# mLSTM attention with a mixture of experts: fades spread by a product and an exponential instead of a stored copy and transfers

## What is computed

```
m_new = max(f_gate[t] + m, i_gate[t])
f = exp(f_gate[t] + m - m_new);  i = exp(i_gate[t] - m_new);  m = m_new
C = f * C + i * outer(v[t], k[t]);   n = f * n + i * k[t]
y[t] = sigmoid(o_gate[t]) * (C @ q[t]) / max(|n . q[t]|, 1)
```

## Time and profile before

| | us |
|---|---|
| median of three runs (407.35 to 410.41) | 407.49 |
| the profiled execution, measured from outside | 407.79 |
| its span, from the first to the last instruction | 406.1 |
| TensorE busy | 374.9 |
| VectorE busy | 238.7 |
| ScalarE busy | 220.7 |
| GpSimd busy | 78.6 |

### The profile page before, as it was taken

The page is one execution under the profiler, slowest core; times in us unless marked ns, Lnnn a source line. Parts: engine busy times, 40 slices in busy tenths (PEclk is TensorE's granted clock), DMA queues, the critical chain, the costliest instruction groups (busy, mean ns, idle before and its releaser), DMA issues.

```text
span 406.1 us, 9533 instructions
## 1 busy us (share of the span) xinstructions
PE 374.9 (92%) x3484; PEld 315.6 (78%) x3484; DVE 238.7 (59%) x556; ACT 220.7 (54%) x436; POOL 78.6 (19%) x119
## 2 busy tenths in 40 slices
PE   2989978898799879999999999999999999999996
PEld 2667756576667657634569999999999999999996
DVE  8745756745856576441158756556556556556553
ACT  3554546455546565312048866666666666666662
POOL 4255645354544544000000000000000000000000
PEclk9996999998989999999999999999999999999999
DMA  6389999999999998996900001001001001001001
GB/s 179 90 245 254 268 283 254 243 263 265 260 260 241 254 257 283 350 363 217 364 6 2 0 2 65 2 2 65 0 0 65 0 0 65 0 0 65 0 2 65
DMA packets 31816, 56.83 MB, mean 140 GB/s; under 512 B 3524, under 2 KB 20548, under 8 KB 31524
## 3 DMA queue, kind: packets, MB, share of 16 engines
q1 hardware_dynamic: 28308, 45.84, 40.5%
q10 hardware_dynamic: 3472, 10.51, 9.6%
HBM read 51.83 MB, written 4.42 MB: 139 GB/s over the span
## 4 chain that ended last, share of the span: by engine, by line
PE 68%; DMA 13%; SPq 11%; DVE 4%; issue 2%; ACT 1%; ACTq 0%; DVEq 0%
DMA row_x<-cum_scratch 12%; PE heads_banks L1109 7%; PE high_banks L1111 7%; PE high_banks L1110 7%; PE high_banks L1109 7%; PE heads_banks L1110 7%; PE heads_banks L1111 7%; PE low_banks L1097 5%; SPq L393 3%; PE low_banks L1032 2%; PE heads_banks L823 2%; PE low_banks L802 2%; PE low_banks L1013 2%; PE low_banks L959 2%; SPq L351 2%
## 5 line engine op out<-in xcount | busy, mean ns | idle before, releaser
L747 ACT ACTIVATE relu_h<-low_banks 128x512 f32<-128x512 f32 x96 | 57.4, 598 | 60.5 <-PE low_banks L1097 60.1
L1422 DVE CAST sq_hi<-sq_h 128x512 fp32r<-128x512 f32 x96 | 41.0, 427 | 66.7 <-ACT sq_h L752 66.1
L1424 DVE TENSOR_TENSOR sq_lo<-sq_h,sq_hi 128x512 fp32r<-128x512 f32 x96 | 66.5, 692 | 3.3
L752 ACT ACTIVATE sq_h<-relu_h 128x512 f32<-128x512 f32 x96 | 60.6, 632 | 3.1
L1111 PE MATMUL high_banks<-wo_hi,sq_lo 128*128 128x320 f32 x192 | 59.3, 309 | 0.0
L1109 PE MATMUL high_banks<-wo_hi,sq_hi 128*128 128x320 f32 x192 | 59.3, 309 | 0.0
L1110 PE MATMUL high_banks<-wo_lo,sq_hi 128*128 128x320 f32 x192 | 59.3, 309 | 0.0
L1109 PE MATMUL heads_banks<-wo_hi,sq_hi 128*128 128x320 f32 x192 | 59.3, 309 | 0.0
L1110 PE MATMUL heads_banks<-wo_lo,sq_hi 128*128 128x320 f32 x192 | 59.1, 308 | 0.0
L1111 PE MATMUL heads_banks<-wo_hi,sq_lo 128*128 128x320 f32 x192 | 59.1, 308 | 0.0
L1152 DVE TENSOR_TENSOR att_w<-low_banks,att_w 128x512 f32<-128x512 f32 x48 | 30.9, 685 | 37.2 <-POOL att_w L538 21.0
(11 more groups left out here) (177 smaller groups left out, 548.8 us busy)
## 6 DMA issues: line engine op xcount, KB each, us to landing
w_sb<-in_w SPq DMA_DIRECT2D x8, 1280.0 KB, 12.5
w_a<-in_w ACTq DMA_DIRECT2D x16, 512.0 KB, 9.6
kv_in<-in_kv SPq DMA_DIRECT2D x24, 320.0 KB, 13.8
qk_in<-in_qk SPq DMA_DIRECT2D x24, 256.0 KB, 7.2
fade_b<-fade_scratch SPq DMA_DIRECT2D x40, 128.0 KB, 8.3
o_in<-in_o_gate SPq DMA_DIRECT2D x24, 160.0 KB, 13.6
out<-out_sb SPq DMA_DIRECT2D x5, 640.0 KB, 3.2
wo_raw<-in_w_out SPq DMA_DIRECT2D x4, 640.0 KB, 12.0
```

The source lines that it names most:

```text
L747: act.activation(relu_h[:, slot], bank[slot][:, :], ACT.Relu).then_inc(relu_done, 1)
L752: act.activation(sq_h[:, slot], relu_h[:, slot], ACT.Square).then_inc(sq_done, 1)
L1422: dve.tensor_copy(sq_hi[:, slot], sq_h[:, slot]).then_inc(hi_done, 1)
L1424: dve.tensor_tensor(sq_lo[:, slot], sq_h[:, slot], sq_hi[:, slot].bitcast(F32), ALU.subtract).then_inc(lo_done, 1)
```

## The change

The fades are no longer stored and loaded. A constant matrix `cum_pick` (42 x 128, zeros and ones) is made at the start by GpSimd with a memset and two selects. In each step, `spread_fade` on TensorE multiplies it with the 42 rows of `row_x`: it picks the high and the low row of `cum` for each group of heads and writes their sum to the 64 partitions of the group, 4 x 128 values each, in bank 1. `raise_fade` on ScalarE takes the exponential from there into `fade_b`. The readers wait for `fade_ready` in place of a transfer. Because bank 1 is used once more, the second decay product and `logit` wait for the exponential, and `spread_fade` waits for the decay exponentials of its step. `load_rows` also waits until the product four steps back has read its row. On GpSimd `mask` now stands ahead of `scale_q`. The exponential at the start, its tile and the scratch tensor are gone.

```diff
--- before.py
+++ after.py
@@ -104,6 +104,7 @@
         slot_sum = sb("slot_sum", [TS, 1])
         slot_twice = sb("slot_twice", [TS, P])
         row_half = sb("row_half", [P, KC + 1])
+        cum_pick = sb("cum_pick", [QUAD + H + 2, 2, DP], F32R)
 
 
         with ExitStack() as own:
@@ -118,7 +119,6 @@
             f_plus_m = src
             keyw_log = sb("keyw_log", [NS, S], stack=own)
             keyw = sb("keyw", [NS, S], stack=own)
-            fade = sb("fade", [NS, S], stack=own)
             cum_parts = sb("cum_parts", [NS, 2, S], F32R, stack=own)
             src_parts = sb("src_parts", [NS, 2, S], F32R, stack=own)
         with ExitStack() as own:
@@ -207,7 +207,6 @@
 
         cum_dram = nc.dram_tensor("cum_scratch", [NS, 2, S], F32, kind="Internal").ap()
         src_dram = nc.dram_tensor("src_scratch", [NS, 2, S], F32, kind="Internal").ap()
-        fade_dram = nc.dram_tensor("fade_scratch", [B, NC, H * L], F32, kind="Internal").ap()
 
 
         consts_in = sem("consts_in")
@@ -218,7 +217,6 @@
         rows_stored = sem("rows_stored")
         rows_direct = sem("rows_direct")
         src_loaded = [sem(f"src_loaded{i}") for i in range(2)]
-        fades_loaded = [sem(f"fades_loaded{i}") for i in range(FADE_RING)]
         qk_loaded = [sem(f"qk_loaded{i}") for i in range(3)]
         kv_loaded = [sem(f"kv_loaded{i}") for i in range(3)]
         o_loaded = [sem(f"o_loaded{i}") for i in range(3)]
@@ -244,6 +242,10 @@
         scores = sem("scores")
         weights = sem("weights")
         log_i_ready = sem("log_i_ready")
+        pick_made = sem("pick_made")
+        pick_placed = sem("pick_placed")
+        fade_logs = sem("fade_logs")
+        fade_ready = sem("fade_ready")
         q_scaled = sem("q_scaled")
         kw_ready = sem("kw_ready")
         v_ready = sem("v_ready")
@@ -313,7 +315,7 @@
 
 
         G_START, G_M, G_FM, G_LOGF, G_CUM, G_SRC, G_CUMLO, G_SRCLO, G_KEYW = range(1, 10)
-        A_CUM, A_FADE, A_SRC, A_KEYW = range(1, 5)
+        A_CUM, A_SRC, A_KEYW = range(1, 4)
 
         decay_bank, score_bank = bank[0:2], bank[2:4]
         merge_bank, heads_bank, turned_bank, side_bank = bank[4], bank[5], bank[6], bank[7]
@@ -322,6 +324,7 @@
         state_ps = side_bank[:, 0:HP * DP].rearrange("p (j e) -> p j e", j=HP)
         xT_ps = bank[0][:, 0:KC * L].rearrange("p (k t) -> p k t", k=KC)
         logit_ps = bank[1][0:TS, 0:L]
+        fade_ps = bank[1].rearrange("p (j t) -> p j t", j=HP)
         turn_ps = side_bank[:, 0:NC * NS].rearrange("p (c s) -> p c s", c=NC)
         comb_ps = side_bank[:, 0:3 * P]
 
@@ -377,25 +380,12 @@
             def load_rows(b, c):
                 n, s = step(b, c), step(b, c) % ROW_RING
                 at_least(sp, decay_logs, 2 * (n - ROW_RING + 1))
+                at_least(sp, fade_logs, rescales(*before(b, c, ROW_RING)))
                 t0 = c * L
                 for r in range(2):
                     rows = cum_dram[H * b + HP * r:H * b + HP * (r + 1), :, t0:t0 + L].rearrange("h k t -> k h t")
                     p0 = QUAD * r + H
                     sp.dma_start(row_x[p0:p0 + 2, :, s].bitcast(F32), rows).then_inc(rows_loaded[s], 16)
-
-            def load_fades(b, c):
-                s = fade_slot(b, c)
-                at_least(sp, q_scaled, rescales(b, c) - FADE_RING)
-                pb, pc = (b, c - FADE_RING) if c > FADE_RING else (b - 1, c - FADE_RING + NC - 1)
-                at_least(sp, carry_half, (NC - 2) * pb + min(pc, NC - 2))
-                for r in range(2):
-                    row = fade_dram[b, c:c + 1, HP * L * r:HP * L * (r + 1)]
-                    sp.dma_start(fade_b[DP * r:DP * (r + 1), s].rearrange("p h t -> p (h t)"), row.broadcast_to([DP, HP * L]))\
-                        .then_inc(fades_loaded[s], 16)
-
-            def store_fades(b):
-                to = fade_dram[b].rearrange("c (h t) -> h c t", h=H)
-                sp.dma_start(to, fade[H * b:H * (b + 1), :].rearrange("h (c t) -> h c t", t=L)).then_inc(rows_stored, 16)
 
             def load_src(b):
                 at_least(sp, decay_logs, 2 * NC * (b - 1))
@@ -430,16 +420,10 @@
             direct_cum(0)
             sp.wait_ge(gate_vec, G_CUMLO)
             direct_cum(1)
-            sp.wait_ge(gate_act, A_FADE)
-            store_fades(0)
             sp.wait_ge(gate_act, A_SRC)
             direct_src(sp, 0, 0)
             sp.wait_ge(gate_vec, G_SRCLO)
             direct_src(sp, 1, 0)
-            sp.wait_ge(rows_stored, 16)
-            load_fades(0, 1)
-            for b in range(1, B):
-                store_fades(b)
             sp.dma_start(cum_dram, cum_parts[:, :, :].bitcast(F32)).then_inc(rows_stored, 16)
             sp.dma_start(src_dram, src_parts[:, :, :].bitcast(F32)).then_inc(rows_stored, 16)
             sp.wait_ge(cleared, 3)
@@ -448,9 +432,7 @@
             load_o(0, 1)
             sp.dma_start(phi_sb[:, 0:2], phi[0:2 * P, :].rearrange("(k p) s -> p k s", p=P)).then_inc(phi_loaded, 16)
             sp.dma_start(phi_sb[0:DM_LAST, 2], phi[2 * P:DM, :]).then_inc(phi_loaded, 16)
-            sp.wait_ge(rows_stored, 16 * (B + 2))
-            load_fades(0, 2)
-            load_fades(0, 3)
+            sp.wait_ge(rows_stored, 32)
             sp.wait_ge(keyw_turned, 1)
             sp.wait_ge(rows_direct, 96)
 
@@ -463,8 +445,6 @@
                     load_kv(*far)
                     if step(*far) >= ROW_RING:
                         load_rows(*far)
-                    if far[1] > 0 and far != (0, 3):
-                        load_fades(*far)
                     load_qk(sp, *far)
                 if n + 2 < STEPS:
                     load_o(*after(*after(b, c)))
@@ -525,7 +505,7 @@
 
             def scale_q(b, c):
                 s = c % 2
-                pool.wait_ge(fades_loaded[fade_slot(b, c)], 32 * ((rescales(b, c) - 1) // FADE_RING + 1))
+                pool.wait_ge(fade_ready, rescales(b, c))
                 pool.wait_ge(qk_loaded[c % 3], 32 * (step(b, c) // 3 + 1))
                 at_least(pool, heads, step(b, c) - 1)
                 pool.tensor_tensor(q_fade[:, s], qk_in[:, c % 3, 0], fade_b[:, fade_slot(b, c)], ALU.mult).then_inc(q_scaled, 1)
@@ -545,6 +525,12 @@
             pool.memset(qk_in[:, 2], 0.0).then_inc(cleared, 1)
             pool.memset(k_w[:, :, :, :], 0.0).then_inc(cleared, 1)
             pool.memset(carry[:, :, :, :], 0.0).then_inc(cleared, 1)
+            pool.memset(cum_pick[:, :, :].bitcast(F32), 1.0).then_inc(pick_made, 1)
+            for side in range(2):
+                pool.wait_ge(pick_made, side + 1)
+                pool.affine_select(out=cum_pick[:, :, :], in_=cum_pick[:, :, :].bitcast(F32), compare_op=ALU.is_ge, fill=0.0,
+                                   base=(-H, H + 1)[side], pattern=[[(-QUAD, QUAD)[side], 2], [0, DP]],
+                                   channel_multiplier=(1, -1)[side]).then_inc((pick_made, pick_placed)[side], 1)
 
             mask(0, 0)
             pool.wait_ge(cleared, 4)
@@ -558,9 +544,9 @@
                 b, c = n // NC, n % NC
                 if c < NC - 1:
                     weigh_keys(b, c)
+                mask(b, c)
                 if c > 0:
                     scale_q(b, c)
-                mask(b, c)
 
 
 
@@ -587,6 +573,14 @@
                                    decay_bank[r][:, :].rearrange("p (h t) -> p h t", h=HP), ACT.Exp)\
                         .then_inc(decay_exp, 1)
 
+            def raise_fade(b, c):
+
+                act.wait_ge(fade_logs, rescales(b, c))
+                at_least(act, q_scaled, rescales(b, c) - FADE_RING)
+                pb, pc = (b, c - FADE_RING) if c > FADE_RING else (b - 1, c - FADE_RING + NC - 1)
+                at_least(act, carry_half, (NC - 2) * pb + min(pc, NC - 2))
+                act.activation(fade_b[:, fade_slot(b, c)], fade_ps, ACT.Exp).then_inc(fade_ready, 1)
+
             def copy_v(b, c):
                 act.wait_ge(kv_loaded[c % 3], 16 * (step(b, c) // 3 + 1) if isinstance(b, int) else 32 * b + 16 * (c // 3 + 1))
                 at_least(act, heads_turned, step(b, c) - 1)
@@ -615,7 +609,7 @@
             def load_w1(n):
                 if n == 1:
                     act.wait_ge(rows_direct, 96)
-                    act.wait_ge(rows_stored, 16 * (B + 2))
+                    act.wait_ge(rows_stored, 32)
                     act.wait_ge(keyw_turned, 1)
                 if n % 5 > 0 and n - n // 5 <= len(W1_PARTS):
                     e, k = W1_PARTS[n - n // 5 - 1]
@@ -661,7 +655,6 @@
             act.activation(row_x[0:QUAD + H], ring, ACT.Copy).then_inc(rows_one_hot, 1)
             act.wait_ge(gate_vec, G_CUM)
             act.activation(cum_parts[:, 0], cum[:, :], ACT.Copy).then_inc(gate_act, 1)
-            act.activation(fade[:, :], cum[:, :], ACT.Exp).then_inc(gate_act, 1)
             act.wait_ge(gate_vec, G_SRC)
             act.activation(src_parts[:, 0], src[:, :], ACT.Copy).then_inc(gate_act, 1)
             act.wait_ge(rows_fixed, 1)
@@ -684,6 +677,8 @@
```

(19 more changed lines are left out.)

## The result

The changed kernel takes 391.86 us (median of four runs, 391.69 to 392.09), the kernel before 408.95 (median of four, 407.35 to 410.79): a ratio of 0.958, interval 0.953 to 0.963. That is faster, by 17.1 us against the median of four and 15.6 against that of the first three. I had forecast 398.0 and a range of 388 to 406. The profiled execution took 392.09 us outside, with a span of 390.4, against 407.79 and 406.1.

A forecast was written before the change was run, and what follows sets the result against it. Transfers were taken to pace the attention loop, TensorE some 10% behind. Work 115.7, products 6.0, bank 1.0, idle 5.4 and transfer waits 2.0 made 130.1 against 139.3; with the start 9.5 less, 398.0 us, range 388 to 406.

The forecast's parts named there:

- The transfers' new time: Attention loop: without 5.2 MB of fade loads, 31.0 MB remain, 119 us at the same 260 GB/s.
- Removed issues and SP's wait: SP's queue: two issues a step and the carry_faded wait go, unpriced in the loop; 0.3 us gained at the start.
- The product: TensorE: 20 added products at 0.3 us each, 6.0 us, within bounds of 0 to 9.9.
- The exponential at no cost: ScalarE: 20 added exponentials of 0.6 us fit in the wait before copy_xT, costing nothing; uncovered, 12 us.
- Rival 3: Shared bank serialises: ScalarE's exponential delays every decay, +11.7 us, 419; chance 0.09.
- The bank: TensorE at the shared bank: spread_fade waits for the decay exponential in chunk 1's case, four times, 1.0 us.
- Mask ahead of `scale_q` at nothing: GpSimd: scale_q, now behind the mask, still ends 1.4 us before attend reads q_fade; nothing counted.
- The idle time: TensorE in the loop: 5.4 us of other idle left, plus 2.0 of left-over transfer waits.
- The clock: TensorE in the loop: three low-clock stretches cost some 6.0 us, which goes, leaving 115.7 of work.
- Rival 4: TensorE's clock: 20 more short waits on PSUM keep it lower more often, +7 us, 414; chance 0.04.
- Rival 1: Full relief: transfers pace the loop to the end at 119 us, products nearly all hidden, 387.5; chance 0.15.
- Rival 2: Only the named transfer waits go; clock dips stay, products cost the full 0.5 us each, 406; chance 0.17.

The follow-up runs named there:

- idle_full: The changed kernel plus two unread 128 KB loads a step at the old place in SP's order, behind the old waits: 407.29 us, ratio 0.999.
- before_small: The kernel before with each fade load reading 16 of 512 columns, same issues and waits, output not the reference's: 391.60 us, ratio 0.963.
- idle_small: The changed kernel plus two unread 4 KB loads a step at the old place, behind the old waits: 392.87 us, ratio 0.966.
- two_products: The changed kernel with each fade product issued twice in a row into the same place: 397.06 us, ratio 0.976.
- before_swap: The kernel before with only GpSimd's order changed, mask ahead of scale_q: 407.98 us, ratio 1.001.
- old_order: The changed kernel with GpSimd's old order, scale_q ahead of mask: 403.97 us, ratio 0.993.
- idle_half: The changed kernel plus two unread 64 KB loads a step at the old place, behind the old waits: 393.82 us, ratio 0.967.

## Why the prediction was right, and its sizes too small

**The bound: right.** Transfers paced the loop. It is shown from both sides: the bytes put back take the gain away (idle_full), and the bytes taken from the kernel before give it (before_small).

**The transfers' new time: not tested as an end.** I had 119 us at 260 GB/s for what is left. The loop takes 123.06 with TensorE full, at a DMA share of 0.83, so the transfers are no longer the bound.

**Removed issues and SP's wait: right to leave unpriced in the loop.** idle_small has both and costs 1.0 by the medians and nothing in the loop. That `load_qk` would be freer was wrong: it waits 26.7 us for `q_scaled`, and the loop doesn't feel it. At the start I took 0.3 for the store ahead of row_y: the second decay product came 0.1 earlier. What I did not see is that the four stores and the first fade loads stood ahead of the loads of queries and keys as well; the earlier trace rows show only the first of the stores. Against before_small, which keeps them, the step from the fourth to the fifth decay product is 8.30 - 4.88 = 3.4 us shorter, the dip of the clock in it included. In the kernel before it took 9.91; the other 1.6 are what the bytes added on top.

**The product: mis-sized, 6.0 for 4.4 to 5.2.** The timeline shows 0.50 us for each of them, with the next instruction starting 0.01 later; the step gets longer by 0.23. So my sign of being wrong, over 0.4 us of TensorE's time, was ill chosen: the row has more than that and the price is half of it. The price stands in the row of the score behind it, 1.38 us in the step shown, against this one in the step of the earlier trace rows:

```profile
122.73 1.16 PE L802 MATMUL low_banks<-qk_in 64*128 64x128 f32 x16
```

That is 0.22 more (and the score's 16 products took 1.16, not the 1.09 that I had given them). The 19 products of the loop make 4.4 by the steps, all twenty 4.6, or 5.2 by two_products. My estimate from sixteen 128-column products, 0.27, was right to a few hundredths, and the rounding to 0.3 was not needed. By the Trainium skill (TensorE: Matmul & The Clock Gate, "Back-to-back issue gap") an isolated 512-column product takes 216 ns, which would have made 4.3 us; the measured 0.22 to 0.26 lie just above it.

**The exponential at no cost: right.** ScalarE's wait before `copy_xT` went from 0.85 to 6.4 / 18 = 0.36 us, where I had named about 0.5 as its sign, and a second exponential costs 0.09 each. What the first one costs by itself no run isolates. Rival 3 fell: the cover did not shrink to nothing, and it decided nothing.

**The bank: 1.0 where 0.4 was.** `spread_fade` waited twice, for 0.2 us each (its weight load 1.2 in three cases, most of it beside other products). My 0.25 for each of four cases was near; they were fewer.

**Mask ahead of `scale_q` at nothing: right for the time, wrong for the reason.** I had judged the order by the slack of the new one and never costed the old one in the new kernel. By itself the order is worth nothing (before_swap), but without it the change would give 0.7% and not 4.2% (old_order).

**The idle time: the largest miss.** I kept 5.4 us of other idle, 1.0 at the bank and 2.0 of left-over transfer waits, 8.4 together; 4.4 were left. The 2.0 failed outright: at a share of 0.83 there were no transfer waits at all, where I had worked with 0.92 and bursts. And of the 6.4 of idle that named no transfer I had counted 1.0 as going, with the masks; with 4.4 left, 0.4 of it at the bank, 2.4 went. Of these, 1.3 stood at `attend` waiting for `weigh` (1.6 us, 0.3 now). That they were the transfers' too, by way of loads that came late on ScalarE's or GpSimd's side, is my reading and not isolated.

**The clock: right, as a part of the gain.** I gave 6.0 us of 121.67 to the stretches at a lower clock. The busy time is now 118.64 at a granted clock of 1.00, of which 4.4 are the 19 products of the loop at 0.23 each: 114.3 of old work, 1.4 under my 115.7. Rival 4 fell; 20 more users of a bank leave the clock at 1.00 over the loop, and in idle_full it is 0.96 where the transfer waits come back. Idle time alone does not bring the dips: in old_order TensorE is idle for 13.8 of the loop's 133.5 us, in waits of at most 0.9, and the clock is 1.00; the kernel before has 17.6, in waits of up to 1.7, and 0.95. The Trainium skill (the same page, "A second HAM failure mode: psum-queue depth-cycling") tells of a kernel in which the clock swings between its levels because TensorE idles briefly between groups of products while it cycles through PSUM banks; this case's trace does not show that.

In numbers, the loop that I added up to 130.1 is 123.06: 1.4 less work, 1.6 less for the products, 4.0 less idle, 7.0 in all. Rival 1, with 119, was closer than my forecast, and the measured time lies in its range; but its mechanism is not what happened. Transfers do not set the pace (a share of 0.83), and the products are not hidden (0.23 each). It failed at TensorE's work, as I had said, but I had put too much on top. Rival 2, in which only the named waits go, fell: the clock came back too.

**The same gain by another way.** 139.26 to 123.39 by the bytes alone; then 3.4 less for the start and 4.4 more for the products, which leaves 1.3 less, for which I see the collision of q_fade and carry_faded: TensorE's waits for the carry behind it, 0.7 and 0.7 us, are about that much. But old_order has waits for the carry too, 1.7 us, with carry_faded at 0.32, so this last share is argued and not isolated.

## What to carry over

Where a stretch shows a DMA share of 1 and the engine that waits names a transfer of 4 KB, look for the bytes in front of it and not for the issues: a queue that waits for a consumer can be a symptom; here it waited longer in the faster kernel. And count the recovery whole: with the transfer waits go the clock dips that they bring and, here, 2.4 us of idle time put down to other engines. When a value that was loaded far ahead is now computed in the step, go through every in-order queue that reads it and move what does not need it ahead; that order may be worth nothing before and most of the gain after.

## What the runs showed of the hardware

- **The time does not follow the bytes in proportion.** Half of 5.24 MB back costs 2.0 us by the medians (the share is 0.94 in its one trace, of an execution 4.8 us longer than the median), all of it 15.4 (share 0.99).
- **The same 10.51 MB of weights take less of the engines when these are less full.** The row of their queue (packets, MB, share of 16 engines over the span), before and after:

```profile
q10 hardware_dynamic: 3472, 10.51, 9.6%
```

```profile
q10 hardware_dynamic: 3472, 10.51, 7.8%
```

  9.6% of 406.1 us is 39.0 us of all engines, 7.8% of 390.4 is 30.5: a packet's time seems to hold waiting too, so a share near 1 says that the engines are occupied and not what they could move. The row varies: the other traces without the fade bytes have 7.6 to 8.4%, idle_half 8.9 and the two others with all bytes 9.6 and 9.7. That the difference is waiting is my reading of the same packets taking longer.
- **GpSimd beside VectorE.** carry_faded takes 0.32 to 0.33 us with nothing on GpSimd beside it, and 1.35 when it starts 0.11 behind q_fade (95.94 us in before_small, q_fade from 95.83 to 97.10). The mask slows VectorE too, but less: x_odd takes 0.99 us for two beside it (60.83 in the changed kernel) and 0.55 with nothing beside it (72.82). `weigh`, which reads the scores from PSUM, is not slowed by q_fade: 0.68 us each at 63.47 and 64.07 in the changed kernel, with q_fade from 63.22 to 64.69, and 0.69 at 46.95 with nothing beside it.
